# The first block of a gated scan turned by TensorE instead of VectorE, its halves of d_model as even and odd columns

## What is computed

```python
sig = 1.0 / (1.0 + np.exp(-f_logit))
f = lower_bound + (1.0 - lower_bound) * sig          # lower_bound has 256 values
h = f[:, t] * h + (1 - f[:, t]) * x[:, t]            # y[:, t] = h
...
x = (np.maximum(y @ w_in1, 0) ** 2) @ w_out1         # 256 -> 2048 -> 256
h = x @ w_in2
out = np.where(h > 0, h, np.exp(np.minimum(h, 0)) - 1) @ w_out2
```

## Time and profile before

| | |
|---|---|
| median of 3 runs | 1985.73 us (1984.5 to 1987.32) |
| the profiled execution's own time | 1983.23 us |
| its span, first to last instruction | 1981.4 us |
| mean granted clock of TensorE | 0.998 |
| busy: TensorE, VectorE, ScalarE, GpSimd | 99%, 80%, 76%, 31% |
| time until the products with w_out begin | 32.07 us |

### The profile page before, as it was taken

The page is one execution under the profiler, slowest core; times in us unless marked ns, Lnnn a source line. Parts: engine busy times, 40 slices in busy tenths (PEclk is TensorE's granted clock), DMA queues, the critical chain, the costliest instruction groups (busy, mean ns, idle before and its releaser), DMA issues.

```text
span 1981.4 us, 27907 instructions
## 1 busy us (share of the span) xinstructions
PE 1963.1 (99%) x8714; PEld 1634.4 (82%) x8714; DVE 1579.0 (80%) x1769; ACT 1511.1 (76%) x1816; POOL 608.6 (31%) x505
## 2 busy tenths in 40 slices
PE   7999999999999999999999999999999999999998
PEld 5887888888888888888888888888888888889888
DVE  6646888888788888888888888878888887866887
ACT  6887777778778787777877777777777787777766
POOL 3355323223232232332323323223232232322410
PEclk9999999999999999999999999999999999999999
DMA  6679544444444444344444444435444343443453
GB/s 165 195 212 258 157 140 125 146 144 132 130 136 139 126 146 146 115 143 136 129 136 146 135 128 139 137 109 156 146 125 142 136 125 117 146 127 122 139 173 111
DMA packets 251784, 283.08 MB, mean 143 GB/s; under 512 B 178952, under 2 KB 188168, under 8 KB 251656
## 3 DMA queue, kind: packets, MB, share of 16 engines
q1 hardware_dynamic: 247424, 280.76, 46.8%
q10 hardware_dynamic: 4232, 0.98, 0.3%
HBM read 249.30 MB, written 32.37 MB: 142 GB/s over the span
## 4 chain that ended last, share of the span: by engine, by line
PE 95%; ACT 2%; SPq 1%; DMA 1%; DVE 1%; issue 0%; POOL 0%; ACTq 0%; DVEq 0%
PE acc L576 51%; PE ring L576 44%; DMA lb<-in_lower_bound_dram 0%; SPq L393 0%; SPq L340 0%; DMA o_sb<-in_moe_w_in_dram 0%; ACT xb L930 0%; ACT xa L930 0%; ACT xa L928 0%; DVE y_raw L1395 0%; ACT xb L928 0%; ACT hid_hi L994 0%; ACT t_hi L1060 0%; DVE y_raw L1387 0%; ACTq L1044 0%
## 5 line engine op out<-in xcount | busy, mean ns | idle before, releaser
L576 PE MATMUL acc<-hid_hi,wout 128*128 128x512 f32 (+1 forms) x3072 | 1142.0, 387 | 0.0
L576 PE MATMUL ring<-t_hi,s_w 128*128 128x512 f32 (+1 forms) x2720 | 1036.5, 388 | 12.0 <-DVE t_lo L1401 10.3
L576 PEld LDWEIGHTS acc<-hid_hi,wout 128*128 128x128 f32 x3072 | 576.8, 188 | 113.3
L576 PEld LDWEIGHTS ring<-t_hi,s_w 128*128 128x128 f32 x2720 | 511.2, 188 | 115.9 <-DVE s_w L1219 7.2
L576 PE MATMUL acc<-hid_lo,wout 128*128 128x512 f32 (+1 forms) x1536 | 594.7, 387 | 0.0
L576 PE MATMUL ring<-t_lo,s_w 128*128 128x512 f32 (+1 forms) x1360 | 527.0, 388 | 0.0
L1646 POOL TENSOR_TENSOR xb<-xb,m_sb 128x512 f32<-128x512 f32 (+1 forms) x176 | 225.9, 1283 | 965.7 <-DVE hid_lo L1309 961.2
L1005 ACT ACTIVATE m_sb<-ring 128x512 f32<-128x512 f32 (+1 forms) x176 | 104.5, 594 | 363.4 <-PE ring L576 340.1
L576 PEld LDWEIGHTS acc<-hid_lo,wout 128*128 128x128 f32 x1536 | 288.4, 188 | 56.6
L576 PEld LDWEIGHTS ring<-t_lo,s_w 128*128 128x128 f32 x1360 | 255.7, 188 | 50.5
L1309 DVE TENSOR_TENSOR hid_lo<-xa,hid_hi 128x1024 fp32r<-128x1024 f32 (+1 forms) x191 | 231.3, 1211 | 81.4 <-ACT hid_hi L984 81.3
(11 more groups left out here) (111 smaller groups left out, 1701.7 us busy)
## 6 DMA issues: line engine op xcount, KB each, us to landing
s_w<-s_kept SPq DMA_DIRECT2D x184, 512.0 KB, 3.8
s_w<-s_kept SPq DMA_DIRECT2D x176, 384.0 KB, 4.1
wout<-w_kept SPq DMA_DIRECT2D x96, 512.0 KB, 4.4
out_dram<-o_sb SPq DMA_DIRECT2D x88, 128.0 KB, 3.5
f_raw<-in_f_logit_dram SPq DMA_DIRECT2D x168, 64.0 KB, 3.6
x_raw<-in_x_dram SPq DMA_DIRECT2D x168, 64.0 KB, 2.8
s_kept<-ee SPq DMA_DIRECT2D x16, 512.0 KB, 3.8
s_kept<-s_w SPq DMA_DIRECT2D x8, 512.0 KB, 4.0
```

Source lines behind the costliest of these rows:

```text
L576: mm = nc.tensor.matmul(out_ap, lhs[a], rhs[b], start=start and t == 0, stop=stop and t == 2)
```

## The change

Block 0's rows are loaded whole: one DMA for each batch and tensor (`load_first`), with step k * 128 + p on partition p. TensorE turns them by 128 x 128 transposes with an identity, f into `acc[:, 1]` and x into `acc[:, 0]`, four for each half. The identity is a memset by VectorE and one `affine_select` by GpSimd. The two halves of d_model are now the even and the odd columns, everywhere: VectorE's turns of the later blocks read every second column, and w_in1's rows are loaded by the same rule, in two DMAs a pair. lower_bound is one row of 256 values, second on SP's queue, turned by two small transposes. tanh, gates and products are made half by half and read `acc` directly, so VectorE's four turns of block 0 are gone. The 26 matmuls on zeros become 8 ahead of the transposes of batch 1 and 16 behind them. `up` is cut into halves: pair 0's and pair 1's products of half 0, batch 1, stand ahead of the transposes of batch 0's f and x, and all products of one half come before those of the other. On ScalarE and VectorE w_in's split of pair 1 and a few splits change places.

The core of the diff:

```diff
 BI = {(0, 0): 0, (1, 0): 1, (1, 1): 2, (0, 1): 3}
 RING = 4
-WARM = 26
+WARM = (8, 16)
 NP = 7
 NQ = 4
 NS = 4
...
+        lb_row = lb_sb[0:1, :]
+        lb = ring[:, RING - 1, 0:CH]
+        f_turn = acc[:, 1]
+        x_turn = acc[:, 0]
+        def load_first(eng, src, b, dst, loaded):
+            o = dst[:, b].rearrange("p n s -> p (n s)").rearrange("p (k d) -> p k d", d=D)
+            eng.dma_start(o, src[b, 0:S, :].rearrange("(k p) d -> p k d", p=P)).then_inc(loaded[b], DMA_INC)
...
         @block.sync
         def _(sp):
-            win1_v = w_in1.rearrange("(a c e) (k f m) -> a e c k f m", a=G, c=CH, f=2, m=P)
+            win1_v = w_in1.rearrange("(p c) (k f m) -> p c k f m", c=CH, f=2, m=P)
             win2_v = w_in2.rearrange("(c p) (k f m) -> p c k f m", p=P, f=2, m=P)
...
                         load_w2(pair_of(ph, p))
-            load_rows(f_logit, 1, 0, S, xa[:, 1].rearrange("p n s -> p (n s)"), f0_loaded[1], range(2))
-            load_rows(x, 1, 0, S, xb[:, 1].rearrange("p n s -> p (n s)"), x0_loaded[1], range(2))
+            load_first(sp, f_logit, 1, xa, f0_loaded)
+            sp.dma_start(lb_row, lower_bound.rearrange("(o d) -> o d", o=1)).then_inc(lb_loaded, DMA_INC)
             load_raw_in(1, 0)
-            load_rows(f_logit, 0, 0, S, xa[:, 0].rearrange("p n s -> p (n s)"), f0_loaded[0])
             load_raw_in(1, 1)
-            load_rows(x, 0, 0, S, xb[:, 0].rearrange("p n s -> p (n s)"), x0_loaded[0])
+            load_first(sp, x, 0, xb, x0_loaded)
             load_raw_out(1, 0)
             load_raw_in(1, 2)
             load_f(1, 0)
...
                 elif pr.g > 2:
                     pe.wait_ge(relu_n1 if n else relu_n0, pr.g)
+            def up_half(pr, n, c):
+                v = pr.phase.order % 2
                 o = plain_banks(pr, n)
+                for f in range(2):
+                    mm = triple(o[:, f], [s_w[:, pr.par(), QI[f, c], h, :] for h in range(2)],
+                                [t[v][:, BI[c, n], :] for t in (t_hi, t_lo)], c == 0, c == 1)
+                if c == 1:
+                    mm.then_inc(up_n1 if n else up_n0, 1)
+            def up(pr, n):
+                up_ready(pr, n)
                 for c in range(CH):
-                    if pr.g == 0:
-                        pe.wait_ge(y0_lo, CH * (1 - n) + c + 1)
-                    for f in range(2):
-                        mm = triple(o[:, f], [s_w[:, pr.par(), QI[f, c], h, :] for h in range(2)],
-                                    [t[v][:, BI[c, n], :] for t in (t_hi, t_lo)], c == 0, c == 1)
-                mm.then_inc(up_n1 if n else up_n0, 1)
+                    up_half(pr, n, c)
             def down(pr, k, c):
...
                     up(pair_of(ph, p), 1)
                     up(pair_of(ph, p), 0)
+            def warm(n):
+                for t in range(n):
+                    nc.tensor.matmul(ring[:, t % 2, :], zeros[:, 0:P], zeros[:, 0:BANK], start=True, stop=True)
+            def turn(b, src, dst, loaded, read, turned):
+                rows = src[:, b].rearrange("p n s -> p (n s)").rearrange("p (k e c) -> p k c e", e=P, c=CH)
+                pe.wait_ge(loaded[b], DMA_INC)
+                for c in range(CH):
+                    if b == 0:
+                        pe.wait_ge(read, c + 1)
+                    for k in range(S // P):
+                        mm = nc.tensor.transpose(dst[:, c, k * P:(k + 1) * P], rows[:, k, c], ident)
+                    mm.then_inc(turned, 1)
+            pr0, pr1 = pair_of(first(0), 0), pair_of(first(0), 1)
             pe.wait_ge(zeros_in, 1)
-            for t in range(WARM):
-                nc.tensor.matmul(acc[:, t % 2, 0, :], zeros[:, 0:P], zeros[:, 0:BANK], start=True, stop=True)
-            for n in (1, 0):
-                for p in range(2):
-                    up(pair_of(first(0), p), n)
+            warm(WARM[0])
+            pe.wait_ge(ident_done, 1)
+            turn(1, xa, f_turn, f0_loaded, None, f0_turned)
+            pe.wait_ge(lb_loaded, DMA_INC)
+            for c in range(CH):
+                mm = nc.tensor.transpose(lb[:, c:c + 1], lb_row.rearrange("o (e c) -> o c e", c=CH)[:, c], ident[0:1, 0:1])
+            mm.then_inc(lb_turned, 1)
+            turn(1, xb, x_turn, x0_loaded, None, x0_turned)
+            warm(WARM[1])
+            pe.wait_ge(y0_lo, 1)
+            up_ready(pr0, 1)
+            up_half(pr0, 1, 0)
+            turn(0, xa, f_turn, f0_loaded, tanh0_done, f0_turned)
+            pe.wait_ge(consts_done, 2)
+            up_ready(pr1, 1)
+            up_half(pr1, 1, 0)
+            turn(0, xb, x_turn, x0_loaded, x0_gated, x0_turned)
+            pe.wait_ge(y0_lo, 2)
+            up_half(pr0, 1, 1)
+            up_half(pr1, 1, 1)
+            for c in range(CH):
+                pe.wait_ge(y0_lo, CH + c + 1)
+                for pr in (pr0, pr1):
+                    if c == 0:
+                        up_ready(pr, 0)
+                    up_half(pr, 0, c)
             plain_phase(first(0))
             plain_phase(first(1))
...
             def gates0(b):
-                act.wait_ge(f0_turned, 2 - b)
-                nc.scalar.activation(z_raw[:, :, b, :], z_raw[:, :, b, :], ACT.Tanh, scale=0.5).then_inc(tanh0_done, 1)
-                act.wait_ge(tanh0_done, 2 - b)
-                if b == 1:
-                    act.wait_ge(consts_done, 2)
                 for c in range(CH):
-                    nc.scalar.activation(z_raw[:, c, b, :], z_raw[:, c, b, :], ACT.Identity, scale=amp[:, c:c + 1],
+                    v = CH * (1 - b) + c
+                    t = z_raw[:, c, b, :]
+                    act.wait_ge(f0_turned, v + 1)
+                    nc.scalar.activation(t, f_turn[:, c, :], ACT.Tanh, scale=0.5).then_inc(tanh0_done, 1)
+                    act.wait_ge(tanh0_done, v + 1)
+                    if v == 0:
+                        act.wait_ge(consts_done, 2)
+                    nc.scalar.activation(t, t, ACT.Identity, scale=amp[:, c:c + 1],
                                          bias=mid[:, c:c + 1]).then_inc(gates0_done, 1)
             def split0(b, c):
                 act.wait_ge(scanned0, CH * (1 - b) + c + 1)
                 nc.scalar.activation(t_hi[0][:, BI[c, b], :], y_raw[:, c, b, :], ACT.Copy).then_inc(y0_hi, 1)
-            load0(f_logit, 1, xa[:, 1], f0_loaded[1], range(2, G))
-            load0(x, 1, xb[:, 1], x0_loaded[1], range(2, G))
-            with nc.allow_non_contiguous_dma(reason="256 values"):
-                lb_v = lower_bound.rearrange("(a c e) -> c a e", a=G, c=CH)
-                for c in range(CH):
-                    act.dma_start(lb[:, c:c + 1], lb_v[c]).then_inc(lb_loaded, DMA_INC)
+            load_first(act, x, 1, xb, x0_loaded)
+            load_first(act, f_logit, 0, xa, f0_loaded)
             act.wait_ge(carried, 1)
             nc.scalar.activation(x_t[:, 0, 0:CH * B], carry[:, :, :, 0], ACT.Tanh)
             gates0(1)
             quarters_hi(1, 0)
             split0(1, 0)
+            quarters_hi(1, 1)
             split0(1, 1)
-            quarters_hi(1, 1)
             gates0(0)
             pr0, pr1 = pair_of(first(0), 0), pair_of(first(0), 1)
-            plain_act(pr0, 1)
+            plain_relu(pr0, 1)
             split0(0, 0)
+            plain_square(pr0, 1)
+            plain_relu(pr1, 1)
+            split0(0, 1)
             hi_of_n1(pr0)
-            plain_act(pr1, 1)
-            split0(0, 1)
+            plain_square(pr1, 1)
             hi_of_n1(pr1)
             weights_hi_out(1, 0)
             plain_act(pr0, 0)
...
                 return nc.vector.transpose(dst.rearrange("p c (k e) -> p c k e", e=SQ),
-                                           raw[:, 0:n * CH].rearrange("p (k c e) -> p c k e", c=CH, e=SQ))
+                                           raw[:, 0:n * CH].rearrange("p (k e c) -> p c k e", c=CH, e=SQ))
             def turn_f(i, q):
                 n = pieces_of(i)[q][2]
...
-            def turn0(b, raw, dst, loaded, done):
-                dve.wait_ge(loaded[b], G * DMA_INC)
-                turn(raw[:, b].rearrange("p n s -> p (n s)"), dst[:, :, b, :], S).then_inc(done, 1)
             def gate0(b, c):
                 v = CH * (1 - b) + c
                 dve.wait_ge(gates0_done, v + 1)
-                dve.wait_ge(x0_turned, 2 - b)
+                dve.wait_ge(x0_turned, v + 1)
                 nc.vector.scalar_tensor_tensor(out=y_raw[:, c, b, :], in0=z_raw[:, c, b, :], scalar=1.0,
-                                               in1=y_raw[:, c, b, :], op0=ALU.subtract,
-                                               op1=ALU.mult).then_inc(x0_gated, 1)
+                                               in1=x_turn[:, c, :], op0=ALU.subtract, op1=ALU.mult).then_inc(x0_gated, 1)
             def scan0(b, c):
                 v = CH * (1 - b) + c
...
                                         ALU.subtract).then_inc(y0_lo, 1)
             nc.vector.memset(m1_sb[:, 0:HALF], 0.0).then_inc(zeros_in, 1)
```

(20 more changed lines are left out.)

37 lines of the change are left out of this document (17 added, 20 removed).

## The result

The changed kernel has a median of 1981.26 us in 19 runs: 18 lie from 1979.65 to 1982.68, and one run of 4045.54 stands apart and is left out of the ratio. The kernel before, measured beside it, has 1985.4 us in 19 runs (1983.22 to 1987.52). The ratio is 0.998, with a 95% interval of 0.9973 to 0.9986. That is 4.1 us less, small but clear of no change, where 2.5 were forecast.

What follows compares the result with a forecast made beforehand. TensorE, 99% busy, was taken as bound by its late start: L + 34T + W + 17.0 - 34.8 gave 2.5 us earlier, 1983.2 us from a median of 1985.73; range 1979.8 to 1987.2.

Steps and rivals of the forecast that it cites:

- ScalarE's 13 instructions: ScalarE's row from first relu to the end of pair 0, batch 0's high part: 11.4 us forecast, 12.30 before.
- S: Start of the second half of TensorE's first step (pair 0, batch 0): 32.3 us forecast, 34.79 before.
- L: Moment when f of batch 1 has landed at the start: taken as 5.43 us, as before.
- rival 3: Loads come later: L 6.4, gain 1.5 us (1984.2); or clock not risen after 8 matmuls, about +1.5 (1987.2); chance 0.15.
- T: Time of one 128x128 transpose on TensorE: taken as 0.14 us, 34 of them in the sum.
- W: Time of the 16 warming matmuls behind batch 1's transposes: 5.15 us if the clock falls, 3.47 if not.
- The gap ahead of w_out: New TensorE wait of 1 to 2 us before the first products with w_out, near 29 us; none before.
- A shift of this moment is a shift of the end.: Claim that moving S moves the kernel's end equally, since TensorE is fed from there on; 2.5 us earlier forecast.
- R: TensorE's restart near 190 us, behind a wait for ScalarE's m_sb; the prediction gave it no term.
- Rival 1: Transposes keep TensorE's clock up, W is 3.47: gain 3.9 us (1981.8), up to 5.5 (1980.2); chance 0.30.
- Rival 2: f32 transposes on TensorE are slow, T 0.227 to 0.426: from 1.2 us faster to 7.3 slower; chance 0.14.
- Rival 4: The start is not what counts, so nothing is gained: 1985.7 us; chance 0.03.

Runs made afterwards that it cites:

- the repetition of after: The changed kernel run again unedited, with a second profile: 1981.05 us, ratio 0.9979 to the kernel before, span 1979.0.
- a4: Changed kernel with f and x of batch 1 each loaded in halves over both queues, f first: 1979.14 us, ratio 0.9969 to the kernel before.
- a2_warm8_0: Changed kernel without its second row of warming matmuls (0 for 16): 1983.84 us, ratio 0.9993 to the kernel before.
- a7: a4 with pair 0's products ahead of pair 1's on TensorE and lower_bound's transposes between the halves of f's: 1977.87 us, ratio 0.9966 to before.
- a5: a4 with w_out's pair 0 split one step earlier on ScalarE and VectorE: 1978.44 us, ratio 0.9968 to the kernel before.
- a3_turns_warm: Changed kernel with 24 transposes of the identity in place of the 16 warming matmuls: 1981.04 us, ratio 0.9981 to the kernel before.

## Why the prediction was right, and where it was off

The time (1981.26) lies within 1979.8 to 1987.2, and the chain named was the right one: first product, first relu, ScalarE's 13 instructions, low part, S. But the range is wide and takes in the time of before itself, and the forecast time of 1983.2 was 1.9 us too high, by three terms and a baseline. It also held the gain for too small to be told from none; with 19 runs on each side it is told.

**The baseline.** It was said that the profiled execution is 2.5 below the median and that the same 2.5 may be taken for both kernels. This step failed. The first profile of before has its clock back at 18.9 us, two others at 24.3, with S at 36.3 and 36.4. The changed kernel stands idle hardly at all ahead of its products and does not pay this. Profile against profile, the first of before and the repetition of after differ by 2.4 us (spans) and 2.30 (S); the other 1.7 of the 4.1 is about what the late clock cost the two other profiles of before at S (1.5 and 1.6). That is of the size of the 1.3 us that 50 warming matmuls gave the kernel of before, and the 2.9 us by which the changed kernel is still ahead of that one are of the size of the 2.4. It rests on three profiles of before and is no more exact than that.

**L, the landing of f** (5.43 taken, 6.4 in rival 3): 6.54 and 6.40, rival 3's value. Two whole 512 KB loads side by side take 5.6 and 6.1 us from issue to landing, against 2.7 and 3.8 in the earlier trace rows. The bound from above named 6.4 too, but from two errors that cancel: bytes from 2 us on at 236 GB/s, where they came from 3.0 us on at up to 386. This cost 1.1 us, and a4 won it back and more.

**T, a transpose** (0.14 taken): 0.12 to 0.13 us at full clock, better than taken. At half clock it is 0.21 to 0.235, and the first 18 ran at half in both profiles of the changed kernel: 3.98 us from 6.57 to 10.55, where 2.52 were forecast. The step that failed here is that the clock has risen once the 8 matmuls are over, which the earlier trace rows had shown only once, in a row of 26. It does rise in time in some executions, as in a2_warm8_0. Rival 3 had the other case, at +1.5.

**W, the 16** (5.15 taken, 3.47 if the clock stays up): 4.31 us in the first profile, 3.26 in the repetition, 3.9 in a7. The reason given was wrong: the clock did not rise and fall, it rose late, at the end of the transposes in the repetition and among the 16 in the first profile.

In the first profile these make 14.86 - 13.10 = 1.76 us: 1.14 (start of f's turns) + 1.46 (T) - 0.84 (W). In the repetition, 13.63: 1.00 + 1.42 - 1.89 = 0.53. That the forecast first product was only 0.53 off there is luck: two terms 2.4 us too small and one 1.9 too large.

**From the first product to the relu** 6.52 were forecast: 6.48 and 6.44. **ScalarE's 13 instructions**, 11.4: 11.10, with no wait for TensorE. **The low part**, 1.3: 1.32. Thus S = 32.3 + 1.76 - 0.04 - 0.3 = 33.7, measured 33.76. **The gap ahead of w_out**, 1 to 2 us near 29: 1.33 at 30.72. A second wait at S, 0.48, was not foreseen.

**What was set at nothing:** the identity takes 0.29 us on GpSimd and was covered by 4.8; the strided turns cost 1 ns of 693; w_in held nothing up at the start of the changed kernel. lower_bound was nearly free but not quite: the gates wait 0.91 us for it, because its transposes stand behind all eight of f's (in a7, where four stand ahead of them, this wait is gone).

**"A shift of this moment is a shift of the end."** True behind R, to 0.03 us, but for the second fall of the clock (1.64). Between S and R it holds to 1.4 (156.7 to 158.1 us), by the w_in load near 180 us, which took back all 0.8 in a5.

**The rivals.** Rival 1 was half right: no fall, but in the changed kernel's profiles no early rise either. Rival 2 fell (T 0.12). Rival 3's two parts both came true in the profile. Rival 4 is excluded by the interval.

## What to carry to other kernels

Take a few profiles of the same kernel before sizing an edit of 0.1 to 0.2%: here one program's spans lay 3.3 us apart, and the spacing of weight loads told why at a glance. When a long wait is removed, look for the load that lands next: lower_bound alone gave nothing, the whole change 4 us, and who goes first among the loads another 2. Idle TensorE time ahead of a burst cost twice here, once as a wait and once as the slow clock behind it (1.5 us at S in the kernel before, 2.8 us in a2_warm8_0).

## What was not expected of the hardware

- The moment at which TensorE's clock rises differs between executions of one program: 12.67 and 10.2 us in the changed kernel, 18.9 and 24.3 in the one before, with the same instructions ahead of it.
- f32 transposes of 128x128 are 0.12 to 0.13 us apart at 2.4 GHz and 0.21 to 0.235 at 1.2. In a3_turns_warm the clock came up while only they had run since 6.96, and held. But it was also seen to fall among them once: in a3 f's eight were at full clock from 6.96, behind 2.2 us of waiting, and x's at half from 8.55.
- A wait of 2.18 us in the middle of steady work was followed, 1.5 us after the restart, by 3.4 us at half clock. In a5 one of 2.15 us was not.
- The granted clock of the profile can't be used for the first microseconds. It reads 1.00 in every stretch up to 16 us of the changed kernel, where the loads are 0.43 us apart up to 12.67:

```profile
8.00:12.00 4.00, 4.00 (x17) 1.00 1.12 336
```
